# Attention masks compared from bucket numbers in HBM instead of pattern products on TensorE

## The reference, cut to what matters

```python
q_bits = (einsum('bhsd,dk->bhsk', q, proj) > 0)      # 6 bits a token and head
k_bits = (einsum('bhsd,dk->bhsk', k, proj) > 0)
q_bucket = sum(q_bits * powers); k_bucket = sum(k_bits * powers)   # powers = 1, 2, 4, ... 32
mask = q_bucket[..., :, None] == k_bucket[..., None, :]
scores = where(mask, scale * q @ k.T, -1e9)
attn = exp(scores - max) ; attn = attn / (sum(attn) + 1e-9) ; out = attn @ v
```

## Time and profile before

| What | us |
|---|---|
| median of 3 runs | 746.33 |
| lowest, highest | 744.53, 747.09 |
| the profiled execution's own time | 746.62 |
| its span in the trace | 744.8 |
| pairs 1 to 6, first scores of one to first scores of the next, on average | 28.28 |
| pair 7, first scores to 2.05 behind the scores of its tile 11 (the distance from tile 11 to the next tile 0 elsewhere) | 27.61 |

### The profile page before, as it was taken

How to read it: one execution, slowest core, us unless ns; L and a number is a source line. 1 busy time by engine, 2 the same in 40 slices (tenths; PEclk the granted TensorE clock), 3 DMA queues, 4 the chain that set the end, 5 groups by cost and what they waited for, 6 DMA issues and landing times.

```text
span 744.8 us, 12026 instructions
## 1 busy us (share of the span) xinstructions
PE 704.6 (95%) x3809; PEld 592.4 (80%) x3809; DVE 423.3 (57%) x795; ACT 321.8 (43%) x634; POOL 265.1 (36%) x269
## 2 busy tenths in 40 slices
PE   7789999999999999999999999999974999999995
PEld 3379999999999887888888888888863788778884
DVE  0499999999999855458345646633347411331110
ACT  0087878878878842222211222221414322442221
POOL 0666777777677740035006203600001112112111
PEclk9999999999999999999999999999986999999998
DMA  9922321311341110003001100010117711101010
GB/s 293 255 59 58 99 53 53 105 53 53 96 128 47 57 57 1 0 2 114 0 1 56 56 0 0 1 58 0 57 58 254 258 54 42 44 29 58 28 58 33
DMA packets 22348, 50.80 MB, mean 68 GB/s; under 512 B 3136, under 2 KB 5312, under 8 KB 22304
## 3 DMA queue, kind: packets, MB, share of 16 engines
q1 hardware_dynamic: 19008, 42.34, 17.9%
q0 software_dynamic: 2320, 7.34, 2.9%
q10 hardware_dynamic: 976, 0.56, 0.3%
HBM read 43.95 MB, written 6.55 MB: 68 GB/s over the span
## 4 chain that ended last, share of the span: by engine, by line
PE 88%; DVE 4%; DMA 3%; SPq 1%; issue 1%; ACT 1%; ACTq 0%; POOL 0%; POOLq 0%; DVEq 0%
PE ps L1189 9%; PE ps L1208 8%; PE ps L1353 6%; PE ps L1355 6%; PE ps L1354 6%; PE ps L1335 6%; PE ps L1336 6%; PE ps L1337 6%; PE ps L1222 5%; PE ps L1223 5%; PE ps L1464 3%; PE ps L1466 3%; PE ps L1465 3%; PE ps L1424 3%; PE ps L1426 3%; PE ps L1425 3%
## 5 line engine op out<-in xcount | busy, mean ns | idle before, releaser
L675 ACT ACTIVATE relu<-ps 128x512 f32<-128x512 f32 x48 | 28.7, 598 | 190.6 <-PE ps L1337 190.6
L831 DVE TENSOR_TENSOR pt_lo<-ps,pt_hi 128x384 fp32r<-128x384 f32 x192 | 100.2, 552 | 10.2 <-ACT pt_hi L622 6.3
L622 ACT ACTIVATE pt_hi<-ps 128x384 fp32r<-128x384 f32 x192 | 87.8, 499 | 40.5 <-PE ps L1208 25.5
L611 ACT ACTIVATE probs<-ps,neg_max 128x768 f32<-128x768 f32 x96 | 87.2, 908 | 29.1 <-DVE neg_max L822 28.9
L1208 PE MATMUL ps<-cst,probs 128*128 128x128 f32 x576 | 90.3, 274 | 1.2 <-DVE pt_lo L831 1.1
L822 DVE TENSOR_REDUCE neg_max<-ps 128x1 f32<-128x768 f32 x96 | 90.9, 948 | 0.0
L1353 PE MATMUL ps<-wo_hi,g_hi 128*128 128x512 f32 x192 | 76.0, 396 | 0.6 <-DVE xt_lo L899 0.6
L1355 PE MATMUL ps<-wo_hi,g_lo 128*128 128x512 f32 x192 | 75.5, 393 | 0.0
L1354 PE MATMUL ps<-wo_lo,g_hi 128*128 128x512 f32 x192 | 75.4, 393 | 0.0
L1335 PE MATMUL ps<-xt_hi,wi_hi 128*128 128x512 f32 x192 | 75.1, 391 | 0.0
L1208 PEld LDWEIGHTS ps<-cst,probs 128*128 128x128 f32 x576 | 70.0, 144 | 6.4 <-DVE pt_lo L831 2.1
(11 more groups left out here) (156 smaller groups left out, 1507.7 us busy)
## 6 DMA issues: line engine op xcount, KB each, us to landing
w_raw<-w SPq DMA_DIRECT2D x16, 512.0 KB, 5.5
raw_k<-kT SPq DMA_DIRECT2D x32, 192.0 KB, 3.3
raw_q<-qT SPq DMA_DIRECT2D x32, 192.0 KB, 3.6
wi_raw<-w_in SPq DMA_DIRECT2D x4, 1024.0 KB, 5.0
wo_raw<-w_out SPq DMA_DIRECT2D x4, 1024.0 KB, 5.0
pair_raw<-qT SPq DMA_DIRECT2D x8, 384.0 KB, 7.1
pair_raw<-kT SPq DMA_DIRECT2D x8, 384.0 KB, 13.8
raw_v<-v SPq DMA_DIRECT2D x16, 192.0 KB, 2.4
```

The source lines that it names most:

```text
L831: nc.vector.tensor_tensor(pt_lo[c % 2][sl], unit(tt, h).rearrange("p (k q) -> p k q", k=3), pt_hi[c % 2][sl].bitcast(F32), ALU.subtract).t ...
```

## The change: what it does

`buckets` is a new tensor in HBM, (16 heads, 2, 768) in bf16, with the bucket number of each token. It is made once: VectorE works out column weights from `patt` at its start (`prepare`: a memset, a product of 96x1024, a sum over 96x1024 and a copy, and two small operations that make `lane`, the bucket number that a partition stands for), TensorE multiplies `bits` with them in 3 products for q (in `first_masks(0)`) and 3 for k, VectorE keeps them as bf16 (`keep_ids`), and SP writes them to HBM in three transfers and waits for their landing. For each pair SP then loads the two heads' numbers, one row to all 64 partitions of a half (`load_buckets`), ahead of the pair's other loads, and VectorE makes the whole `mask_st` of the next pair by one comparison of 128x1536 with `lane` (`next_masks`), in iteration `MASK_TILE` = 3 behind `rest_units`. The products of `MASK_TILES` and their six comparisons are gone; those of pair 0 stay. `mask_st` is now 0 or 1 for keys too, so GpSimd scales the query rows by 2^60 and makes the key rows by subtracting ones, as a `tensor_tensor` where a `tensor_scalar` stood.

```diff
...
 PAIRS_BEFORE_HEAD = 2
-MASK_TILES = (2, 3, 5, 6, 8, 9)
-MASK_UNITS = len(MASK_TILES)
+MASK_UNITS = 6
+MASK_TILE = 3
+ID_ROWS = 32
 BACK_TILES = (10, 1, 4, 7)
...
     y_rows = nc.dram_tensor("y_rows", (TOK, DM), F32).ap()
+    buckets = nc.dram_tensor("buckets", (NH, 2, SEQ), BF16).ap()
     with ExitStack() as ctx:
...
             load_v(0, 1, True)
+            sp.wait_ge(ids_kept, 2)
+            for a in range(3):
+                sp.dma_start(buckets[:, :, MASK_W * a:MASK_W * (a + 1)],
+                             bucket_ids[ID_ROWS * a:ID_ROWS * a + NH, :, :]).then_inc(ids_out, 16)
+            sp.wait_ge(ids_out, 48)
+
+            def load_buckets(i):
+
+                sp.wait_ge(masks_staged, i + (MASK_UNITS - 1))
+                for z in range(2):
+                    sp.dma_start(bucket_of[half(z, True), :, :], buckets[ds(i * 2 + z, 1), :, :].to_broadcast(
+                        [HD, 2, SEQ])).then_inc(ids_in, 16)
+
             with sp.Fori(1, PAIRS) as i:
+                load_buckets(i)
                 load_heads(i, False)
...
             def place_masks(i, z):
-                pool.wait_ge(masks_staged, i * MASK_UNITS + MASK_UNITS)
+                pool.wait_ge(masks_staged, i + MASK_UNITS)
                 pool.wait_ge(scores_done, i * TILES_PER_PAIR + (QT * (z + 1) - TILES_PER_PAIR))
                 m = half(z, True)
-                for c, stack in ((0, qb), (1, kb)):
-                    copied(stack[z][m, :], mask_st[m, c, :], 1.0, masks_in, i * 4 + (2 * z + c + 1))
+                copied(qb[z][m, :], mask_st[m, 0, :], BIG, masks_in, i * 4 + (2 * z + 1))
+                hold()
+                G.tensor_tensor(kb[z][m, :], mask_st[m, 1, :], ones_c[m, 0:1].to_broadcast([HD, SEQ]),
+                                ALU.subtract).then_inc(masks_in, 1)
+                pool.wait_ge(masks_in, i * 4 + (2 * z + 2))
             def split_v(i, z, first):
...
                                         ALU.is_gt).then_inc(bits_done, 1)
-            def stage_mask(m, part, dst, src):
+            def first_mask_of(m, part, dst, src):
                 col = MASK_W * (m % 3)
...
                 v_.wait_ge(scores_done, i * TILES_PER_PAIR + (tt + 1))
-                if tt in MASK_TILES and not last:
-
-                    v_.wait_ge(masks_in, i * 4 + 4)
-                    m = MASK_TILES.index(tt)
-                    stage_mask(m, slice(0, P), mask_st[:, m // 3, :], beside(z, MASK_W)).then_inc(masks_staged, 1)
                 if tt in BACK_TILES:
...
                                         negate=True).then_inc(max_done, 1)
+
+            def next_masks(i):
+
+                v_.wait_ge(ids_in, i * 32 + 32)
+                v_.wait_ge(masks_in, i * 4 + 4)
+                nc.vector.tensor_scalar(mask_st[:, :, :], bucket_of[:, :, :], lane[:, :], None,
+                                        ALU.is_equal).then_inc(masks_staged, 1)
             def rest_units(i, tt):
...
                         rest_units(i - 1, TILES_PER_PAIR - 1)
+                    if tt == MASK_TILE and not last_:
+                        next_masks(i)
                     c, r = divmod(tt - 4, CHUNK_TILES)
...
                             invert(i - 1, c + CHUNKS_PER_PAIR)
+            def prepare(ins, count):
+                ins.then_inc(prepared, 1)
+                v_.wait_ge(prepared, count)
+
+            heads = patt[:, :].rearrange("p (h b) -> p h b", b=HD)
+            weighed = x_rows[0:NH * NBITS, 0:2, :, :].rearrange("p a t d -> p (a t d)")[:, 0:NH * HD].rearrange(
+                "p (h b) -> p h b", b=HD)
+            prepare(nc.vector.memset(powers[:, :], 0.0), 1)
+            prepare(nc.vector.tensor_tensor(weighed, heads, iota128[0:NH * NBITS, 0:HD].unsqueeze(1).to_broadcast(
+                [NH * NBITS, NH, HD]), ALU.mult), 2)
+            weights = x_rows[0:NH * NBITS, 2, 0, 0:NH]
+            prepare(nc.vector.tensor_reduce(weights, weighed, AX, ALU.add), 3)
+            prepare(nc.vector.tensor_copy(powers[:, 0:NH], weights), 4)
+            prepare(nc.vector.tensor_scalar(lane_hi[:, :], tokid[:, 0:1], float(HD), -float(HD), ALU.is_gt, ALU.mult), 5)
+            prepare(nc.vector.scalar_tensor_tensor(lane[:, :], tokid[:, 0:1], -1.0, lane_hi[:, :], ALU.add, ALU.add), 6)
+
+            def keep_ids(c):
+                v_.wait_ge(ids_turned, c + 1)
+                nc.vector.tensor_scalar(bucket_ids[:, c, :], ps[0:3 * ID_ROWS, 7 - c, 256:512], 1.0 / 32, None,
+                                        ALU.mult).then_inc(ids_kept, 1)
+
             for c, stack in ((0, qb), (1, kb)):
...
                     keep_bits(m)
+                if c == 0:
+                    keep_ids(c)
                 for z in range(2):
...
                         v_.wait_ge(masks_turned, m + 1)
-                        placed = stage_mask(m, half(z, True), stack[z], first_mask(m))
+                        placed = first_mask_of(m, half(z, True), stack[z], first_mask(m))
                         if z == 1:
...
             tile_max(0, 0, True, False)
+            keep_ids(1)
             pair(0, True, False)
...
             mm = nc.tensor.matmul
-            def masks(i, m, dst):
-
-                return mm(dst, patt[:, ds(i * P, P)],
+            def masks(m, dst):
+
+                return mm(dst, patt[:, 0:P],
                           bits[:, m // 3, MASK_W * (m % 3):MASK_W * (m % 3) + MASK_W], start=True, stop=True)
...
                     pe.wait_ge(masks_staged, 2)
+                    pe.wait_ge(ids_kept, 1)
                 for m in range(3 * c, 3 * c + 3):
                     pe.wait_ge(bits_done, m + 1)
-                    masks(0, m, first_mask(m)).then_inc(masks_turned, 1)
+                    masks(m, first_mask(m)).then_inc(masks_turned, 1)
+                pe.wait_ge(prepared, 4)
+                for a in range(3):
+                    last_mm = mm(ps[ID_ROWS * a:ID_ROWS * (a + 1), 7 - c, 256:512], powers[:, :],
+                                 bits[:, c, MASK_W * a:MASK_W * (a + 1)], start=True, stop=True)
+                last_mm.then_inc(ids_turned, 1)
             pe.wait_ge(projb_in, 16)
...
                 return last_mm
-            def scores(i, tt, first, last):
+            def scores(i, tt, first):
                 z, j = divmod(tt, QT)
...
                         last_mm = mm(bank[:, lo:hi], a[:, P * j:P * j + P], b[:, lo:hi], start=start, stop=not start)
-                if tt in MASK_TILES and not last:
-                    last_mm = masks(i + 1, MASK_TILES.index(tt), beside(tt % 2, MASK_W))
                 if tt in BACK_TILES:
...
                     pe.wait_ge(exp_done, i * TILES_PER_PAIR + (tt + 1))
+                if first and 2 * tt + h == RING - 1:
+                    pe.wait_ge(ids_kept, 2)
                 if not (first and 2 * tt + h < RING):
...
                     if tt < TILES_PER_PAIR - 2:
-                        scores(i, tt + 2, first, last_)
+                        scores(i, tt + 2, first)
                     elif not last_:
-                        scores(i + 1, tt + 2 - TILES_PER_PAIR, False, False)
+                        scores(i + 1, tt + 2 - TILES_PER_PAIR, False)
                     c, part = divmod(tt - 4, CHUNK_TILES)
...
                         turn_xt(1)
-            scores(0, 0, True, False)
-            scores(0, 1, True, False)
+            scores(0, 0, True)
+            scores(0, 1, True)
             pe.wait_ge(masks_staged, MASK_UNITS)
```

More of the change, by code:

```diff
@@ L126, in program @@
         mask_st = sb("mask_st", [P, 2, SEQ], BF16, 2)
+        bucket_of = sb("bucket_of", [P, 2, SEQ], BF16, 2)
+        bucket_ids = sb("bucket_ids", [3 * ID_ROWS, 2, MASK_W], BF16, 2)
+        powers = sb("powers", [NH * NBITS, ID_ROWS], BF16, 2)
+        lane_hi = sb("lane_hi", [P, 1], F32)
+        lane = sb("lane", [P, 1], F32)
         raw_q = [sb(f"raw_q{z}", [P, SEQ], F32) for z in range(2)]
@@ L264, in program @@
         masks_staged = sem("masks_staged")
+        prepared = sem("prepared")
+        ids_turned = sem("ids_turned")
+        ids_kept = sem("ids_kept")
+        ids_out = sem("ids_out")
+        ids_in = sem("ids_in")
         masks_in = sem("masks_in")
```

## The result

| What, us | before | after |
|---|---|---|
| median (13 runs each) | 746.23 | 749.30 |
| lowest, highest | 744.01, 747.83 | 747.41, 751.12 |
| the profiled execution's own time, its span | 746.62, 744.8 | 747.41, 745.6 |
| first scores of pair 0 | 35.54 | 37.69 |
| from there to the first scores of pair 1 | 24.78 | 25.42 |

The ratio is 1.0038, 95% interval 1.0025 to 1.0051: the changed kernel is about 3 us slower, a little more than the 0.3% that was called the limit of what can be told. The forecast was 747.4 in a range of 744.3 to 751.5, so the loss is nearly three times the +1.1 that was forecast, inside the range. The trace shows one gain and two losses. The profiled execution of after is the quickest of its 13 runs, so it shows less of the losses than the median holds.

What follows compares the result with a forecast made beforehand. TensorE was taken to set the pace in pairs 1 to 6, VectorE close behind. +4.3 (start) + 0.3 - 1.0 (pair 0) - 2.5 (pairs) = +1.1 us gave 747.4 against the median, range 744.3 to 751.5.

Steps and rivals of the forecast that it cites:

- Parts 1 to 3: Pairs 1 to 6: mask products leave, new comparison and dearer key rows come; -2.5 us, between -4.0 and about 0.
- Part 2: `next_masks` on VectorE before tile 5's maximum: 0.57 us, costing 0.2 a pair in all, bounds 0 and 1.3.
- The hold: `next_masks` may be held on VectorE until a running GpSimd operation ends; 0.1 us added for it.
- Part 3: GpSimd's key rows by `tensor_tensor`: 1.82 us for 0.83, +1.0 twice a pair, making tile 0's copy 0.1 late.
- Rival B: GpSimd's chain becomes the bound, key rows costing 2.3 or held by VectorE; pair 28.3, +3.6, 750 us; chance 0.18.
- Rival C: Start cheap and the gain from removing the mask products whole: -2.2, 744.1 us; chance 0.10.
- Part 4: `prepare` at the start delays `bits`, TensorE's first masks and the projection: +4.3 us, between +3.0 and +5.8.
- The slack: At the start, third `bits` ended at 22.79, needed about 23.3: all but 0.4 of the +4.1 us is passed on.
- Part 5: Pair 0: `keep_ids(1)` behind the first maximum +0.3; mask comparisons and products leaving the ramp, one comparison coming, -1.0.
- Part 6: Bucket numbers through HBM in pair 0, SP's wait delaying pair 1's loads: taken as 0, +2.5 once in the range.
- Hidden by 1.5, or 2 late: Pair 0: numbers land at 48.5 to 52 us, `next_masks(0)` is due near 50.
- Hidden by 0.8: GpSimd, its heads late, ends its chain near 63.1 us; pair 1's scores come near 63.9.

Runs made afterwards that it cites:

- the tiny comparison: Changed kernel with the comparison cut to 2 of 768 columns in all pairs but the first; 750.18 us in one execution, 27.93 a pair.
- the load order alone: Changed kernel, SP loading head 0 of pair 1 before it waits for the bucket numbers, preparation left at the start; 748.62 us, ratio 1.0039.

## Why the prediction was right, and where its terms were off

**Parts 1 to 3: right in size, -2.3 for -2.5, and the reason of one piece wrong.** The most that could be won was taken from pair 7, 0.67, and 0.25 was given back to the comparison and to GpSimd. Measured 0.38 was kept of it, but the comparison takes nothing in the loop (27.93 with 0.39 of its 0.61 gone). What is kept back belongs to the loop: pair 7 is written out, and that makes its tiles 2.17. The control was not clean. The written-out versions split the 0.67 (28.28 - 27.61): 28.28 - 28.05 = 0.23 is the loop's share, 28.05 - 27.64 = 0.41 the mask products', and 0.03 is left for the comparison and what else pair 7 lacks. The share won, 0.38 to 0.41, is three products of 0.12 that stood in tiles where TensorE set the pace; in the three other tiles the time was not TensorE's to give.

**Part 2: the price right.** 0.61 for 0.57. It was worked out by the cast's bytes (0.99 by its elements); one time of one form does not show that bytes are the reason. The hold stays outside: in after the comparison of pairs 1 to 6 never took more than 0.62. The rule that the prediction took from the Trainium skill, "SBUF — State Buffer", section "Who interferes with whom", is that VectorE in a mode that uses two ports and GpSimd lock each other out for a whole instruction. The 1.84 in the run with the doubled key rows agrees with it, for an operation of the change itself; in which mode the comparison runs, no trace shows.

**Part 3: too dear.** 1.46 in place of 1.82, +0.63 over the copy and not +1.0. In pair 3 of after the key rows are done at 118.33 and the pair's first scores start at 118.83, 0.50 behind; Rival B's condition was not met. The run with the doubled rows shows how little that room is. Rival C, a cheap start and the whole gain, failed on both its halves.

**Part 4: less than forecast in the profiles, +3.1 for +4.3 (it was given as 3.0 to 5.8).** Eight profiles have the start of after (the two of after and six of its variants), two that of before. First scores start at 39.06 on average in the eight and at 36.0 in the two: +3.1. By terms:

- *The chain came as forecast.* From its first memset to `bits` it takes 3.64 and 3.94 us in the two profiles of after and 4.14 on average in the eight (up to 4.74), forecast 4.1. In after one hold shows, on the last operation, which took 0.61 and ended at 24.19, with the GpSimd operation of 23.36 + 0.82 = 24.18.
- *The slack was mis-sized, and this is most of the difference.* The projection of k goes on at 26.67 on average in place of 23.84, 2.8 later, of which 0.3 are the three number products (25.68 to 26.02 in after; forecast 0.6). So 4.1 - 2.5 = 1.6 of the chain were covered and not 0.4. The 0.4 was read from one trace in which the constants had landed late (at 21.61; in the second profile of before at 20.48). TensorE's pause for k, 0.9 to 2.9 us in the six profiles without the preparation there, is what can cover a part of the chain.
- *The clock cost little here.* From there to the first scores it is 12.16 and 12.15 in before and 12.39 on average in the eight (11.67 in after itself, 13.13 at most): +0.2, for which the prediction added nothing and kept 0.5.

The granted clock (third from the end) is lowest behind the longest pauses. The windows from 20 to 30 us for before, the second profile of before, after, the tiny comparison and the doubled key rows, with pauses before the masks of 2.27, 2.86, 3.45, 5.03 and 5.92:

```profile
20.00:30.00 10.00, 7.73 (x21) 3.51 (x20) 3.71 (x10) 0.00 (x0) 6.80 (x6) 0.83 1.04 312
20.00:30.00 10.00, 7.14 (x20) 3.34 (x19) 3.71 (x10) 0.00 (x0) 5.51 (x6) 0.83 1.04 296
20.00:30.00 10.00, 6.55 (x20) 2.78 (x19) 7.48 (x17) 0.00 (x0) 6.73 (x6) 0.83 1.03 327
20.00:30.00 10.00, 4.97 (x15) 2.04 (x14) 8.31 (x17) 0.00 (x0) 8.06 (x7) 0.71 0.99 324
20.00:30.00 10.00, 4.08 (x12) 1.68 (x12) 7.58 (x17) 0.00 (x0) 7.42 (x6) 0.62 1.02 327
```

0.83 over 10 us means a third of them at 1.2 GHz, the lower of the two levels; before has that too. After has another 0.93 from 30 to 40 us, where before has 1.00.

How sure is the 3.1? The two pairs of medians with the preparation at the start and later give 3.1 (1.7 to 4.5) and 4.3 (2.6 to 6.0, 1.0 of it in pair 0). And one more profile has the start of before: that of before with its pairs written out, where k lands earlier and the first scores start at 32.59. With it as a third, the difference of the starts is 4.2. So the forecast's 4.3 is not excluded.

**Part 5: right where nothing covers it.** With the preparation later and the heads first, pair 0 took 24.21 (the same in the version written out) against 24.78 and 24.77: -0.6, forecast -0.7 (-1.0 + 0.3).

**Part 6: the step that failed.** "Hidden by 1.5, or 2 late" and "Hidden by 0.8" became a 0 in the sum. The landing was the wrong row: `bucket_of` lands 3.2 to 5.0 us behind its issue in after (median 3.5), not 2.4, and the loads of the heads queue behind it. The 2.4 was that of `raw_v`; the same page has 3.3 and 3.6 for `raw_k` and `raw_q`, which are the loads that GpSimd waits for. From the end of `keep_ids(1)` at 40.30 to GpSimd's start at 51.89 it took 11.6 us in after, where the forecast had 42.4 to 52, 9.6. Pair 0 took 25.42 and 25.96 in the two profiles of after and 25.87 in the one with only the last pairs written out: 25.75 on average, 1.5 more than the 24.21 with the cover restored. It comes in two shapes, TensorE waiting for GpSimd at pair 1 (1.41 and 1.16 where it shows; in the first profile of after it falls together with 1.2 us of low clock) or VectorE waiting for the numbers (0.2 to 1.8), and with the tiny comparison, which had both a late number and a low clock, it was worse (27.46). The +2.5 kept in the range held it.

**The sum** from profiles is then +3.1 - 0.6 + 1.5 - 2.3 = +1.7, against +3.1 measured (+1.9 to +3.8 by the interval). That the forecast, +1.1 on 746.33, came no further off is luck in part: Part 4 was taken 1.2 too high by these profiles while Part 6 was 1.5 too low. What the last 1.4 us are, stays open. Part 4's size is loose by about as much. Or it is the clock: the mean granted clock over the timed runs is 0.9742 after (13 runs) and 0.9779 before (23 runs, of another experiment), and (1 - clock) x time is 19.4 against 16.5, 2.9 us; with the load order alone and before beside it on the same chip it is 0.9753 and 0.9782, 2.2 us. Where it falls could be seen in profiled executions only, and these differ: after had 0.57 from 38 to 46 us, its second profile 1.00.

## What to carry to other kernels

A last iteration that is written out is no clean control for iterations in a hardware loop: besides the work that it lacks it lacks the loop. A slack read from one trace (who had been ready when) is a sample; take a second profile before crediting it. And where a change sends data through HBM in the ramp, list the loads that queue behind it: here two waits lay side by side, and only with both gone, and the preparation moved out of TensorE's way, did the kernel come out ahead, by 0.2%. An idle time in front of an operation is not its price either: GpSimd's 9.77 us, in a profile where TensorE was late itself, cost TensorE almost nothing.

## What the runs showed of the hardware that was not expected

- **The loop costs 0.23 to 0.29 us a pair.** Six pairs in the loop take 27.90 to 27.93 each, the same instructions written out 27.64; 28.28 and 28.05 without the change. With the change it is a tenth of a microsecond on each of three tiles of twelve (2.25 to 2.27 become 2.17). TensorE shows no pause in either form. Whether the branch or the waits on register values cost it was not tried.
- **Written out, both kernels win some 3 us more than their pairs show** (4.6 against 1.4 before; 0.9912 / 0.9981 = 0.9931, 5.1 us, against 1.7 for the changed one). The profile of the written-out kernel before accounts for it like this: first scores at 32.59 in place of 35.54, pair 0 longer by 1.04, the pairs shorter by 1.35, and a dense block without this stretch of low clock, which before and after both have:

```profile
510.00:520.00 10.00, 10.00 (x50) 8.57 (x50) 2.82 (x10) 0.00 (x0) 0.00 (x0) 0.83 0.00 0
```

  TensorE had no pause between 500 and 530 us. The loop is not what brings it: the second profile of after lacks the stretch too, and so do the profiles of the load order alone, the tiny comparison and the last pairs written out. What brings it, and why the start is earlier, is open.
- **The hold between VectorE and GpSimd** is not for all of an operation's time. The held comparison ended 0.43 behind the end of the GpSimd operation that it met, where it takes 0.61 alone, and the one that was issued 0.20 before such an end took no longer than alone. It works the other way too: in the run with the preparation later, GpSimd's two-input operation, issued at 25.39 while VectorE's product of 1024 elements ran (24.89 to 26.28), took 2.55 in place of 1.80. Short operations are held as well: the last one of the preparation, on one element a partition, took 0.61, 0.77 and 1.75 beside GpSimd in different profiles, where 12 elements took 0.175.
